# A router matrix turned through DRAM, table and gather order changed, hidden activations split in halves, and 17 dummy transposes at the start

## The reference

```python
# 1: attention, batch 4, 8 heads, 576 positions, head width 64, mask by blocks of 64
scores = where(block_i >= block_j, 0.125 * q @ k.T, -1e9)
attn = softmax(scores); x = (attn @ v) -> (2304 tokens, 512)
# 2: gated layer, inner width 1536
x = (sigmoid(x @ w_gate) * (x @ w_val)) @ w_out
# 3: mixture of experts, 8 experts of inner width 1024, the best one for each token
logits = x @ moe2_w_gate                      # (512, 8), the router matrix
e = argmax(logits); g = softmax(logits)[e]
out[token] = g * (relu(x[token] @ w1[e]) @ w2[e])
```

## Time and profile before

| | us |
|---|---|
| median of three runs | 944.52 (938.6 to 947.0) |
| the profiled execution, its own time | 943.85 |
| its span in the trace | 942.2 |
| PE busy | 889.7 (94% of the span) |
| DVE, ACT, POOL busy | 453.8, 298.6, 270.3 |
| mean granted clock of PE, as a share of full speed | 0.983 |

### The profile page before, as it was taken

The page is one execution under the profiler, slowest core; times in us unless marked ns, Lnnn a source line. Parts: engine busy times, 40 slices in busy tenths (PEclk is TensorE's granted clock), DMA queues, the critical chain, the costliest instruction groups (busy, mean ns, idle before and its releaser), DMA issues.

```text
span 942.2 us, 15562 instructions
## 1 busy us (share of the span) xinstructions
PE 889.7 (94%) x5198; PEld 735.7 (78%) x5199; DVE 453.8 (48%) x1041; ACT 298.6 (32%) x674; POOL 270.3 (29%) x258
## 2 busy tenths in 40 slices
PE   7999898999969999999999999999979999989995
PEld 3545444579959999999999998999868888878883
DVE  5767676742125335325433534656473434472251
ACT  4545554542222113113112112224323433452140
POOL 4123335321232111211211211215133434453232
PEclk9999999999999999999999999999979999999998
DMA  4555444532122002002002000134254435482110
GB/s 140 157 160 160 155 155 149 165 109 80 56 88 67 1 1 68 1 1 68 1 1 68 1 1 1 46 112 118 84 196 150 140 126 196 137 281 67 45 45 29
DMA packets 48527, 85.36 MB, mean 91 GB/s; under 512 B 9295, under 2 KB 21583, under 8 KB 48464
## 3 DMA queue, kind: packets, MB, share of 16 engines
q1 hardware_dynamic: 42704, 69.32, 22.7%
q0 software_dynamic: 3360, 10.50, 3.4%
q10 hardware_dynamic: 2400, 4.72, 1.4%
HBM read 70.28 MB, written 14.76 MB: 90 GB/s over the span
## 4 chain that ended last, share of the span: by engine, by line
PE 77%; DMA 7%; DVE 5%; issue 5%; POOL 2%; ACT 1%; SPq 1%; POOLq 1%; DVEq 0%; ACTq 0%
PE bank L1486 22%; PE bank L1488 22%; PE bank L1487 21%; PE bank L1458 3%; PE bank L1419 3%; PE bank L1431 3%; DMA rinv_scratch<-rinv 3%; DMA rwide<-rinv_scratch 2%; PE bank L1628 1%; DVE nmax L1046 1%; DMA woraw<-in_w_out 1%; PE bank L1591 1%; ACT prob L854 1%; DMA out<-orow,scol 1%; POOL wrb L773 1%
## 5 line engine op out<-in xcount | busy, mean ns | idle before, releaser
L1486 PE MATMUL bank<-xh,w1h 128*128 128x384 f32 x576 | 193.7, 336 | 0.0
L1488 PE MATMUL bank<-xh,w1l 128*128 128x384 f32 x576 | 193.1, 335 | 0.0
L1487 PE MATMUL bank<-xl,w1h 128*128 128x384 f32 x576 | 192.8, 335 | 0.0
L723 POOL TENSOR_TENSOR hl<-hraw,hh 128x384 fp32r<-128x384 f32 x72 | 82.6, 1147 | 364.6 <-ACT hh L883 364.6
L1235 DVE TENSOR_TENSOR hraw<-hraw,bank 128x384 f32<-128x384 f32 x72 | 39.9, 554 | 232.4 <-ACT hraw L930 232.1
L1486 PEld LDWEIGHTS bank<-xh,w1h 128*128 128x128 f32 x576 | 108.2, 188 | 2.4
L1487 PEld LDWEIGHTS bank<-xl,w1h 128*128 128x128 f32 x576 | 108.1, 188 | 2.3
L930 ACT ACTIVATE hraw<-bank 128x384 f32<-128x384 f32 x72 | 35.4, 492 | 230.0 <-PE bank L1488 230.0
L1488 PEld LDWEIGHTS bank<-xh,w1l 128*128 128x128 f32 x576 | 108.1, 188 | 0.0
L854 ACT ACTIVATE prob<-bank,nmax 128x576 f32<-128x576 f32 (+2 forms) x144 | 76.0, 529 | 88.4 <-DVE nmax L1046 85.6
L1486 PE MATMUL bank<-woh,hh 128*128 128x512 f32 x216 | 85.2, 394 | 8.9 <-POOL hl L723 8.9
(11 more groups left out here) (200 smaller groups left out, 1398.5 us busy)
## 6 DMA issues: line engine op xcount, KB each, us to landing
stage<-in_we SPq DMA_DIRECT2D x56, 512.0 KB, 3.9
w1raw<-in_w SPq DMA_DIRECT2D x8, 768.0 KB, 4.5
kt<-in_kT SPq DMA_DIRECT2D x16, 288.0 KB, 3.2
qt<-in_qT SPq DMA_DIRECT2D x16, 288.0 KB, 3.6
rwide<-rinv_scratch SPq DMA_DIRECT2D x32, 144.0 KB, 3.0
xt_scratch<-xo SPq DMA_DIRECT2D x16, 288.0 KB, 2.2
xraw<-xt_scratch SPq DMA_DIRECT2D x6, 768.0 KB, 4.9
y_scratch<-yrow ACTq DMA_DIRECT2D x6, 768.0 KB, 5.0
```

The source lines that it names most:

```text
L723: pool.tensor_tensor(hl[:, f % 2, :], hraw[:, f % 2, :], hh[:, f % 2, :].bitcast(F32), ALU.subtract).then_inc(h_low, 1)
L1486: pe.matmul(out_, wh, ah, start=first, stop=False, skip_group_check=True)
L1487: pe.matmul(out_, wh, al, start=False, stop=False, skip_group_check=True)
L1488: return pe.matmul(out_, wl, ah, start=False, stop=last, skip_group_check=True)
```

## The change

It has six parts. (1) ACT issues, ahead of stage 2, one DMA that writes the router matrix turned round into DRAM (`wrt_dram`, element by element), and SP broadcasts it from there to all partitions in one transfer in step 8 of group 0. The quarters, POOL's turns and the waits on them are gone. (2) PE makes 17 transposes of the identity before the first scores. Nothing reads them. (3) `second_column` and `row_table` stand ahead of `hidden_low(0)` on DVE, and `table(G_LAST)` ahead of two pieces of `expert_up(1)` on PE. (4) POOL's `weights_low` for the second load (two pieces) stands behind `gather(2)`, `gather(3)`, `scatter` and `columns(1)`. SP's last four pieces of that load wait for the transposes of tile 2. (5) The hidden activations go from PE to ACT to DVE and back in halves of four transposes. (6) The gather of tile 0 stands two steps later in the last group.

```diff
@@ tables of steps
-        ROWS0_STEP, GATHER1_STEP = 9, 10
+        GATHER0_STEP, ROWS0_STEP, GATHER1_STEP = 3, 9, 10
-        WRB_STEP = 7
-        WD = D // 4
+        WRB_STEP = 8
@@ SP: loads of w_out in group 0
-                if WRB_STEP <= k < WRB_STEP + 4:
-                    j = k - WRB_STEP
-                    if j:
-                        sp.wait_ge(wrb_made, j)
-                    sp.dma_start(yrow[:].rearrange("p m d -> p (m d)")[:, 0:WD * E],
-                                 wr[j * WD:(j + 1) * WD, :].rearrange("(a d) e -> a (d e)", a=1).to_broadcast([P, WD * E])
+                if k == WRB_STEP:
+                    sp.wait_ge(wrt_stored, 16)
+                    sp.dma_start(wrb[:].rearrange("p e d -> p (e d)"),
+                                 wrt_dram.rearrange("(a e) d -> a (e d)", a=1).to_broadcast([P, E * D])
                                  ).then_inc(wrb_loaded, 16)
@@ SP: load(1), k == 4
-                            sp.wait_ge(el1_done, 2)
+                            sp.wait_ge(ygT_done, 3)
@@ POOL
-            def wrb_turn(j):
-
-                pool.wait_ge(wrb_loaded, 16 * (j + 1))
-                pool.tensor_copy(wrb[:, :, j * WD:(j + 1) * WD],
-                                 yrow[:].rearrange("p m d -> p (m d)")[:, 0:WD * E].rearrange("p (d e) -> p e d", e=E)
-                                 ).then_inc(wrb_made, 1)
...
-                    if G == 0 and WRB_STEP < f <= WRB_STEP + 4:
-                        wrb_turn(f - WRB_STEP - 1)
                     if G == G_LAST:
-                        if f == 1:
+                        if f == GATHER0_STEP:
                             early_gather(0)
...
             gather(2)
-            weights_low(pool, 1, 1, LOW_POOL[:2], ew_low_p)
             pool.wait_ge(tables, 1)
             columns(0)
             gather_ahead(1)
             scatter(1)
             pool.wait_ge(out_stored, 16)
             columns(1)
+            weights_low(pool, 1, 1, LOW_POOL[:2], ew_low_p)
@@ ACT
+            act.dma_start(wrt_dram, wr.rearrange("d e -> e d"), allow_slow_non_contiguous=True).then_inc(wrt_stored, 16)
             for G in range(NG):
                 group(G)
...
-                act.wait_ge(hT_done, t + 1)
...
-                act.copy(hTh[:].rearrange("p c n -> p (c n)"), bank[1][:].rearrange("p a n -> p (a n)")
-                         ).then_inc(hT_high, 1)
+                for half in range(2):
+                    act.wait_ge(hT_done, 2 * t + 1 + half)
+                    act.copy(hTh[:, 4 * half:4 * half + 4, :].rearrange("p c n -> p (c n)"), bank[1][:, half, :]
+                             ).then_inc(hT_high, 1)
@@ DVE (hidden_low is split in the same way)
             dve.sem_inc(orow_done, 1)
+            dve.sem_inc(hT_low, 1)
+            second_column()
+            row_table()
             hidden_low(0)
-            row_table()
             load_table()
@@ PE
             pe.wait_ge(ident_ready, 1)
+            for i in range(17):
+                pe.transpose(pT_psum(0)[:, 0:P], ident[:], ident[:])
...
-                last.then_inc(hT_done, 1)
+                    if c % 4 == 3:
+                        last.then_inc(hT_done, 1)
@@ expert_down
-                pe.wait_ge(hT_high, t1)
-                pe.wait_ge(hT_low, t1)
...
                 for c in range(HC):
+                    if c % 4 == 0:
+                        pe.wait_ge(hT_high, 2 * t1 + c // 4)
+                        pe.wait_ge(hT_low, 2 * t1 + c // 4)
@@ end of stage 2
             turn_hidden(0)
+            table(G_LAST)
             up_half(1, 0, [2, 3])
-            table(G_LAST)
```

More of the change, by code:

```diff
@@ L59, in bass_attention_ffn_moe @@
     rinv_dram = nc.dram_tensor("rinv_scratch", (2, 2, BLK, NB), F32, kind="Internal").ap()
+    wrt_dram = nc.dram_tensor("wrt_scratch", (E, D), F32, kind="Internal").ap()
     y_dram = nc.dram_tensor("y_scratch", (N, D + 1), F32, kind="Internal").ap()
@@ L270, in bass_attention_ffn_moe @@
         wrb_loaded = sem("wrb_loaded")
-        wrb_made = sem("wrb_made")
+        wrt_stored = sem("wrt_stored")
         lg_step = sem("lg_step")
@@ L892, in yout @@
                     act.wait_ge(y_stored, 16 * G)
-                else:
-                    act.wait_ge(wrb_made, 4)
                 for m in range(GM):
@@ L978, in rest @@
                 weights_high(l + 1, 1 - par, range(4 if isinstance(l, int) and l == 0 else 7, 8))
+            act.sem_inc(hT_high, 1)
             rows_high(1)
@@ L988, in _ @@
             act.wait_ge(el1_done, 2)
-            act.wait_ge(hT_done, 1)
+            act.wait_ge(hT_done, 2)
             act.activation(hrow[:, 0:512], bank[0][:, 0, :], ACT.Relu).then_inc(hrow_a, 1)
@@ L1245, in group @@
                         if G == 1 and f == 0:
-                            dve.wait_ge(wrb_made, 4)
+                            dve.wait_ge(wrb_loaded, 16)
                         logit_step, hot_step, _, slot_step, tab_step = route_steps(G)
@@ L1320, in row_table @@
                 done(dve.tensor_copy(gidx[:], tabv[:, 0, :]))
-                second_column()
                 dve.sem_inc(second_known, 1)
@@ L1352, in hidden_low @@
             def hidden_low(t):
-                dve.wait_ge(hT_high, t + 1)
-                dve.tensor_tensor(hTl[:].rearrange("p c n -> p (c n)"), bank[1][:].rearrange("p a n -> p (a n)"),
-                                  hTh[:].rearrange("p c n -> p (c n)").bitcast(F32), ALU.subtract
-                                  ).then_inc(hT_low, 1)
+                for half in range(2):
+                    c = slice(4 * half, 4 * half + 4)
+                    dve.wait_ge(hT_high, 2 * t + 2 + half)
+                    dve.tensor_tensor(hTl[:, c, :].rearrange("p c n -> p (c n)"), bank[1][:, half, :],
+                                      hTh[:, c, :].rearrange("p c n -> p (c n)").bitcast(F32), ALU.subtract
+                                      ).then_inc(hT_low, 1)
             def hidden(t):
                 dve.wait_ge(el1_done, t + 1)
-                dve.wait_ge(hT_done, t)
+                dve.wait_ge(hT_done, 2 * t)
                 dve.tensor_scalar(hrow[:, 512:], bank[0][:, 1, :], 0.0, None, ALU.max).then_inc(hrow_v, 1)
@@ L1624, in turn_hidden @@
                 else:
-                    pe.wait_ge(hT_high, t)
-                    pe.wait_ge(hT_low, t)
+                    pe.wait_ge(hT_high, 2 * t + 1)
+                    pe.wait_ge(hT_low, 2 * t + 1)
                 for c in range(HC):
```

2 lines of the change are left out of this document (1 added, 1 removed).

## The result

The changed kernel takes **968.80 us** (median of 4 runs, 965.77 to 972.05); the kernel before, on the same chip, 944.18. The ratio is 1.027, 95% interval 1.021 to 1.033: slower by 24.6 us, where 924.5 was forecast. The profiled execution took 972.05 us (span 970.4, mean granted clock 0.966), 28.2 above the one of before.

What follows compares the result with a forecast made beforehand. PE, busy 94% of the span, was taken to bound the kernel, with time only in its idle and half-clock stretches. 1.0 + 9.65 + 5.7 + 3.0 = 19.35 off 943.85 gave 924.5 us, range 917 to 931.

Steps and rivals of the forecast that it cites:

- The router matrix, what takes its place: Group 0: the element-wise DMA delays the first output-weight loads by 0 to 4 us, taken as 0.
- The time of the turning itself: Element-wise DMA ahead of group 0: 4096 elements scaled from the gate row's store, 24.5 us, done by 226.5, no wait.
- Rival (b): Small descriptors or the 2 MB hold the `w_out` loads, 4 us at start, 1 at step 9: 929.5 to 931; chance 0.12.
- rival (d): Slower than before: SP waits at step 8 for the turned matrix; 972 us if turning takes 100 us; chance 0.02.
- Turns removed, 9.65: Group 0: PE's idle time and half clock behind POOL's turns of the router matrix go, 13.83 - 4.18 = 9.65 us.
- The 2 MB broadcast at nothing: Step 8 of group 0: one 2 MB transfer, 14.8 us at most, costed at nothing; up to 1 us without cover.
- Start, 1.0: First scores: 17 identity transposes bring full clock, gain between nothing and 1.3 us, taken as 1.0.
- Tables and tile 2, 5.7: Behind stage 2: `expert_up(2)` gains 7.8 us, tile 4's late gather gives back 2.1 (0 to 4.4), net 5.7.
- Halves, 3.0: Last tile: halves cut PE's idle 3.04 us by 1.4, full clock behind it saves 1.6; 3.0 us in all.
- In every tile but the last: nothing: All other tiles: `hTh` and `hTl` lie beside 24 matmuls, so halves change nothing, one more fixed cost per engine apart.
- Gather of tile 0, nothing: Last group: issued two steps later, read six steps further on, so no gain or cost.

Runs made afterwards that it cites:

- e8: The changed kernel with the router matrix turned by four PE transposes from SBUF, no element-wise DMA: 938.8 us (0.992 of the kernel before).
- e2: The kernel before with the router part (part 1) of the change alone: 969.2 us (1.026).
- e4: The changed kernel with 2048 elements turned one by one and the rest copied as 8 rows, so tokens route otherwise: 947.2 us in one run.
- e5: The changed kernel with the element-wise DMA issued by ACT at the program's start instead of ahead of stage 2: 985.5 us (1.038).
- e10: e8 with the hidden activations passed whole again (part 5 undone): 932.7 us (0.986).
- e9: e8 with PE's last two registers read ahead of the loop over the loads instead of behind it: 937.6 us (0.991).
- e11: e8 with DVE's later low parts waiting for POOL's increment behind the scatter: 936.9 us (0.989).
- e12: e11 with e9's edit and SP's last four pieces of the second load held until tile 3's gather has landed: 928.9 us (0.981).
- e6: The kernel before with part 5 (halves of the hidden activations) alone: 949.5 us (1.007).
- e1: The changed kernel with the router matrix brought in as before (quarters, POOL's turns), all other parts kept: 947.9 us (1.002).

## Why the prediction was wrong

**The router matrix, what takes its place: the failed step.** "if the two queues take turns, it is at most that much later: 0 to 4 us. I take 0, since PE has two `up` steps to do ahead of the first `down`". It was 30.9 us (e8 against the changed kernel). Two errors stand in it. The bound took one load among single elements to be late by its own length; it took 35.6 us to landing, nearly to the end of the element queue. And PE's two `up` steps were taken as cover: they end at 215.84, 8.5 us behind SP's issue. The time of the turning itself was sized from the gate row as 24.5 us and was 38.4, 9.4 ns an element in place of 6.0 (47.0 in e2). With the size as it was, but the loads held as long as the elements run (to 205.3 + 24.5 = 229.8, 13.9 less than measured), the sum would have had some 17 us there and come out near the kernel before; that is an estimate, and e4 speaks against it, where the loads outlasted the elements. Rival (b) had the mechanism, with 4 us for its price; rival (d) looked at the wrong wait: SP at step 8 waited for nothing, because the loads of the first steps had already waited for the same packets. The Trainium skill, "DMA: Bandwidth & Descriptors" (Rules for kernel authors), speaks against a last dim that isn't contiguous; the runs agree, and 4096 elements cost 31 us.

**Turns removed, 9.65:** 9.2 measured (e8 against before, 74.7 and 83.95). Right. The 2 MB broadcast at nothing: right, it landed in 7.3 us.

**Start, 1.0:** the first scores are 1.1 faster, and pair 1 starts only 0.3 earlier, released by ACT's `prob`. Over the profiles pair 1 starts at 13.8 to 15.1 with the dummies (twelve kernels, median 14.6; e5, which moves the elements there, left out) and at 14.8 to 15.8 without (four, median 15.2). That is some 0.3 to 0.6, less than the profiles differ among themselves, and no run has the dummies alone.

**Tables and tile 2, 5.7:** 4.1 to 4.7 in seven of the kernels with it. In e5 and e10 it was 2.6, where the half clock behind tile 3's wait lasted 6.8 us in place of 3.4, in e9 1.1, where the gather of tile 4 was late too, and in e11 5.7, with no half clock there. `sel`, the clock and `expert_up(2)` came as forecast. The prediction had `sel` start first, ahead of the low parts; but POOL's gather starts 0.37 us ahead of `sel` and runs to 685.44, and the low parts follow at 685.46: `sel` was not the first there. That it waited for the gather and the low parts one behind the other fits its 5.45 us; no run tests it. The stall came at the gather of tile 3, not 4: SP's four pieces, issued at 714.24, were costed within tile 4's wait, and meet the gather issued at 716.46. With SP behind that gather 3.4 us more are gained (e12 against e8).

**Halves, 3.0:** 0 at the tail of the changed kernel. The sum left out PE's own sequencer: `[3.04 <-DVE hTl]` of the earlier trace rows had two register loads and the branches right behind it, and these end at the same time. With them moved the 2.9 are there. "In every tile but the last: nothing" was the second wrong step: there the halves move DVE's low parts up to 0.6 us ahead, past POOL's scatter in some kernels and past its low parts in all that lose, and the tiles 12 to 15 take 7.3 us more. By the medians the halves cost some 6 us there (e8 against e10). No rival had it. How the shift becomes 7 us is argued above, not shown.

**Gather of tile 0, nothing:** right; in no profile do its transposes wait.

## What to carry to other kernels

A DMA of single elements is priced by what else wants the DMA engines while it runs, not by when its own result is wanted: look for every load in its window. A small matrix that lies in SBUF is turned on PE for 0.6 us. When an edit shortens work in a loop that has slack, compare the order of starts on the two engines that share a port, not only the sum of times; and before cutting the work named as a releaser, look for what would be released next at the same moment. And look where the profiled execution stands among the others: e6's was the fastest of ten, and lacked the loss that its median has.

## What the runs showed of the hardware

- 4096 elements of 4 bytes from DRAM to DRAM: 38.4 us (9.4 ns each) in the changed kernel, 47.0 in e2; a 256 KB load beside them 35.6 and 40.0 us to landing in place of 2.7. With 2048 of them and a second DMA of 8 rows behind, a load still took 31.5.
- The issue of that second DMA (8 rows of 1 KB, e4) took ACT 12.07 us; the one of the elements ahead of it 1.31.
- The issue of an indirect DMA on POOL takes 1.0 us, and 1.9 to 2.0 when a 128x1024 subtraction on DVE has started 0.1 to 0.2 before it.
- Two 128x1024 subtractions that overlap on POOL and DVE: the one whose recorded start is first takes its own time (POOL 2.4 us in e6, DVE 1.2 in e1), the other 3.4 (DVE in e6) or 3.1 (POOL in e1).
- A semaphore increment that stands behind an indirect DMA in POOL's program is recorded 0.8 us before that DMA's start (e11), and DVE, which waits for it, starts 0.2 before the DMA.
- A multiply-reduce of 128x512 with one operand at a stride of 8 elements takes DVE 1.2 us in place of 0.7.
